# First unit as plain 32-bit products, weight splits one per item behind them, and a chunk's steps over more slots

## The reference

```python
mag = np.sqrt(a_re * a_re + a_im * a_im)
scale = np.minimum(mag, 0.999) / (mag + 1e-06)
for t in range(S):
    S_re, S_im = ar * S_re - ai * S_im + kv, ar * S_im + ai * S_re
    y[:, :, t] = q[:, :, t] @ S_re
x = y as (3072, 384)
h = x @ w_in;  x = (h * clip(h + 3, 0, 6) / 6) @ w_out        # first layer, d_ff 2048
h = x @ w2_in; out = (max(h, 0) + alpha * min(h, 0)) @ w2_out  # second layer
```

## Time and profile before

| | us |
|---|---|
| median of 3 runs (1019.43 to 1021.28) | 1019.67 |
| time of the profiled execution | 1020.87 |
| its span, first to last instruction | 1018.8 |
| PE busy (matmul) | 959.4 |
| DVE busy | 601.2 |
| ACT busy | 490.1 |
| POOL busy | 274.6 |

### The profile page before, as it was taken

How to read it: one execution, slowest core, us unless ns; L and a number is a source line. 1 busy time by engine, 2 the same in 40 slices (tenths; PEclk the granted TensorE clock), 3 DMA queues, 4 the chain that set the end, 5 groups by cost and what they waited for, 6 DMA issues and landing times.

```text
span 1018.8 us, 17268 instructions
## 1 busy us (share of the span) xinstructions
PE 959.4 (94%) x6594; PEld 865.3 (85%) x6594; DVE 601.2 (59%) x1090; ACT 490.1 (48%) x881; POOL 274.6 (27%) x251
## 2 busy tenths in 40 slices
PE   0787988999999999999999999999999999999997
PEld 0687888999999999999999998888888888888886
DVE  6888776768887787868872345452433433334332
ACT  7777757667686766767743443221221222212211
POOL 0012222222222222222222333333333333323332
PEclk9999999999999999999999999999999999999999
DMA  5762333343333333432321701010010010100000
GB/s 165 199 156 72 86 75 82 92 106 83 91 94 80 80 99 81 106 97 70 85 62 28 279 24 55 1 41 23 1 63 0 1 62 1 62 1 1 31 1 32
DMA packets 80931, 70.50 MB, mean 69 GB/s; under 512 B 32592, under 2 KB 78160, under 8 KB 80464
## 3 DMA queue, kind: packets, MB, share of 16 engines
q1 hardware_dynamic: 80208, 68.80, 24.7%
q10 hardware_dynamic: 640, 0.59, 0.2%
HBM read 40.90 MB, written 9.44 MB: 49 GB/s over the span
## 4 chain that ended last, share of the span: by engine, by line
PE 75%; DVE 13%; issue 3%; ACT 3%; SPq 3%; DMA 1%; DVEq 0%; ACTq 0%
PE hp L1188 11%; PE hp L1189 11%; PE op L1188 11%; PE hp L1190 11%; PE op L1189 11%; PE op L1190 11%; PE yp L1176 3%; PE gp L1183 3%; DVE gated L882 2%; DVE t_phase L794 2%; SPq L395 2%; DVE t_fb L822 1%; PE gp L1155 1%; SPq L398 1%; DVE t_fb L828 1%
## 5 line engine op out<-in xcount | busy, mean ns | idle before, releaser
L517 POOL TENSOR_TENSOR g_lo<-gated,g_hi 128x384 fp32r<-128x384 f32 (+2 forms) x240 | 272.4, 1135 | 734.8 <-ACT g_hi L612 734.8
L612 ACT ACTIVATE g_hi<-gated 128x384 fp32r<-128x384 f32 (+2 forms) x240 | 129.9, 541 | 344.6 <-DVE gated L897 284.4
L893 DVE TENSOR_SCALAR gate<-hp,alpha_sb 128x512 f32<-128x512 f32 x96 | 72.1, 751 | 239.9 <-PE hp L1190 239.9
L1188 PE MATMUL hp<-x_hi,wa_hi 128*128 128x384 f32 (+1 forms) x432 | 141.9, 329 | 10.4 <-DVE gated L882 9.2
L1188 PE MATMUL op<-g_hi,wb_hi 128*128 128x384 f32 (+1 forms) x432 | 143.0, 331 | 4.3 <-POOL g_lo L517 4.3
L882 DVE SCALAR_TENSOR_TENSOR gated<-gate,hp 128x384 f32<-128x384 f32 (+1 forms) x144 | 72.9, 506 | 121.2 <-ACT gate L605 121.1
L1190 PE MATMUL hp<-x_hi,wa_lo 128*128 128x384 f32 (+1 forms) x432 | 138.7, 321 | 0.0
L1189 PE MATMUL hp<-x_lo,wa_hi 128*128 128x384 f32 (+1 forms) x432 | 138.7, 321 | 0.0
L1190 PE MATMUL op<-g_hi,wb_lo 128*128 128x384 f32 (+1 forms) x432 | 137.6, 318 | 0.0
L1189 PE MATMUL op<-g_lo,wb_hi 128*128 128x384 f32 (+1 forms) x432 | 137.5, 318 | 0.0
L605 ACT ACTIVATE gate<-hp,half 128x384 f32<-128x384 f32 (+1 forms) x144 | 77.2, 536 | 91.8 <-PE hp L1190 91.7
(11 more groups left out here) (107 smaller groups left out, 1581.6 us busy)
## 6 DMA issues: line engine op xcount, KB each, us to landing
st<-prod SPq DMA_DIRECT2D x92, 145.1 KB, 3.0
a_sb<-a_in SPq DMA_DIRECT2D x24, 288.0 KB, 4.0
qk_sb<-qk_in SPq DMA_DIRECT2D x24, 288.0 KB, 3.6
v_pad<-v_in SPq DMA_DIRECT2D x24, 192.0 KB, 3.8
x_raw<-x SPq DMA_DIRECT2D x6, 768.0 KB, 5.7
out<-out_sb SPq DMA_DIRECT2D x6, 768.0 KB, 4.1
st<-prod SPq DMA_DIRECT2D x96, 32.2 KB, 2.2
wa_raw<-w_in SPq DMA_DIRECT2D x6, 512.0 KB, 6.1
```

What stands on the lines that cost most here:

```text
L517: pool.tensor_tensor(g_lo[:, at, 0:wide], gated[:, at * UT:at * UT + wide], g_hi[:, at, 0:wide].bitcast(F32), ALU.subtract).then_inc(glo_d ...
L612: act.activation(g_hi[:, at, 0:wide], gated[:, at * UT:at * UT + wide], ACT.Copy).then_inc(ghi_done, 1)
L893: dve.tensor_scalar(gate[:, at], hp[:, n % 2, 0:wide], 0.0, alpha_sb[:, m:m + 1], ALU.min, ALU.mult).then_inc(gate_done, 1)
L1188: pe.matmul(acc, lhs[0], rhs[0], start=start, stop=False)
```

## The change

In unit 0 `hidden` and `output` are one plain 32-bit product in place of three in fp32r. They read the landed weights (`wa_raw`, `wb_raw`), `x_raw` (which ACT's `x_high` now writes for chunks 0 and 1) and `gated`. So `high` and `low` are gone for items 0 to 15, and `x_low` for chunks 0 and 1. The 24 splits are one per slot, in slots 3 to 26; a DVE split waits until unit 0 has read its block. The letters of steps and the lengths are new: chunks 2 to 8 have a plan SHORT, with product, mask and output steps in slots of their own, the others a plan LONG, close to the one before; `copy_ends` stands behind `high`, and DVE's `gate1` stands ahead of `forward` where b is not with a.

```diff
-STEPS = {5: (0, 1, 1, 2, 3, 3, 4), 6: (0, 1, 1, 2, 3, 3, 4), 7: (0, 1, 1, 3, 4, 5, 6)}
+SHORT = {6: ("a", "bf", "cdo", "egv", "hij", "kl"), 7: ("a", "bf", "cdo", "egv", "hi", "j", "kl")}
+LONG = {5: ("ab", "cdefg", "ov", "hij", "kl"), 6: ("ab", "cdefg", "ov", "hij", "kl", "")}
-LENGTHS = (7, 6, 7, 7, 6, 6, 7, 5, 5, 5, 6, 5, 5, 6, 5, 5, 6, 5, 5, 6, 5, 6)
+LENGTHS = (6, 6, 6, 6, 7, 7, 7) + 4 * (5, 5, 6) + (5, 6, 6)
-W_EARLY = 8
-W_ITEM = 2
+W_ITEM = 3
-    return range(W_EARLY + W_ITEM * n, min(W_EARLY + W_ITEM * (n + 1), len(W_ORDER)))
+    return range(max(0, n - W_ITEM), min(max(0, n + 1 - W_ITEM), len(W_ORDER)))
...
     # SP
-                if "D" in steps:
+                if "g" in steps:
                     if c1 is not None:
                         stack(c1)
...
     # ACT
-                if "A" in steps:
+                if "a" in steps:
                     if keeps:
                         copy_k(c0, 0)
                     if c1 is not None:
                         waves(c1)
-                        copy_ends(c1)
-                if "B" in steps:
+                if "c" in steps:
                     if keeps:
                         copy_k(c0, 1)
                     if c2 is not None:
                         logs(c2)
...
-                high(n + GSTEP)
+                if n + GSTEP >= MT_FF:
+                    high(n + GSTEP)
+                if "b" in steps and c1 is not None:
+                    copy_ends(c1)
                 for w in splits_at(n):
                     split_w(w)
...
     # DVE
+                if "a" in steps and c1 is not None:
                     phases(c1)
                     fractions(c1)
+                    if "b" in steps:
+                        forward(c1)
+                gate1(n + GSTEP)
+                if "b" in steps and "a" not in steps and c1 is not None:
                     forward(c1)
-                gate1(n + GSTEP)
-                if "B" in steps and c1 is not None:
+                if "c" in steps and c1 is not None:
                     backward(c1)
-                if "C" in steps:
-                    if c1 is not None:
-                        product(c1, 0)
+                if "d" in steps and c1 is not None:
+                    with_qk(c1)
+                if "e" in steps and c1 is not None:
+                    product(c1, 0)
+                if "f" in steps:
                     mask(c0, 0)
                     mask(c0, 1)
-                    if c1 is not None:
-                        product(c1, 1)
+                if "g" in steps and c1 is not None:
+                    product(c1, 1)
...
     # PE
+                    if u == 0:
+                        pe.wait_ge(wa_landed[2 * k + m * P//W_DMA], 16)
+                        mm = pe.matmul(hp[:, n % 2, 0:wide], wa_raw[:, at], x_raw[:, u, k, 0:wide], start=k == 0,
+                                       stop=k == KT_DM - 1)
+                    else:
+                        mm = three(...)
...
+                    if u == 0:
+                        mm = pe.matmul(op[:, j, 0:wide], wb_raw[:, at], gated[:, n % GRING * UT:n % GRING * UT + wide],
+                                       start=m == 0, stop=m == MT_FF - 1)
+                    else:
+                        mm = three(...)
...
-                if "D" in steps:
+                if "o" in steps:
                     outputs(c0)
                     if keeps:
                         new_state(c0)
```

More of the change, by code:

```diff
@@ L74 @@
 B_BLOCKS = [(1, n) for n in range(NWI)]
-W_ORDER = (A_BLOCKS[0] + B_BLOCKS[0:1] + A_BLOCKS[1] + B_BLOCKS[1:4] + A_BLOCKS[2] + B_BLOCKS[4:6] + A_BLOCKS[3]
-           + B_BLOCKS[6:])
-W_EARLY = 8
-W_ITEM = 2
+W_ORDER = [b for q in range(NQ) for b in A_BLOCKS[q] + B_BLOCKS[(0, 1, 3, 6)[q]:(1, 3, 6, NWI)[q]]]
+W_ITEM = 3
 NRP = 12
@@ L120, in places @@
         items = items_of(s)
-        for i, n in enumerate(items):
-            yield ("".join(x for x, at in zip("ABCDEFG", STEPS[len(items)]) if at == i), n, chunk_at(s), chunk_at(s + 1),
+        plan = (SHORT if width(items[-1] // MT_FF) == FIRST * CH else LONG)[len(items)]
+        for steps, n in zip(plan, items):
+            yield (steps, n, chunk_at(s), chunk_at(s + 1),
                    chunk_at(s + 2), chunk_at(s + 3))
@@ L443, in _ @@
                         load_qk(c2)
-                if "F" in steps and c1 is not None:
+                if "j" in steps and c1 is not None:
                     load_v(c1)
-                if "G" in steps:
+                if "k" in steps:
                     c4 = chunk_at(c0 + 4)
@@ L529, in _ @@
                                pattern=[[1, ROWS2]], channel_multiplier=-1).then_inc(masks_set, 1)
-            for n in range(NT):
+            for n in range(MT_FF, NT):
                 low(n)
@@ L598, in x_high @@
                 need(act, h_done, (u - 1) * MT_FF)
[L599 removed]
+                to = x_hi if u > 0 else x_raw
+                act.activation(to[:, u % 2, :, x_cols(c)], y_place(c), ACT.Copy).then_inc(xhi_done, 1)
             def gate_of(n):
@@ L640, in _ @@
             act.wait_ge(consts_set, 1)
[L641 to L645, removed]
             def decay_parts(c):
@@ L679, in _ @@
             x_high(1)
-            split_some(W_EARLY - 4)
             inverses(3)
-            for n in range(2):
-                gate_of(n)
-                high(n)
+            gate_of(0)
+            gate_of(1)
             squares(4)
@@ L707, in _ @@
                         logs(c2)
-                if "D" in steps and c2 is not None:
+                if "v" in steps and c2 is not None:
                     inverses(c2)
-                if "E" in steps:
+                if "h" in steps:
                     x_high(c0)
-                if "F" in steps and c3 is not None:
+                if "j" in steps and c3 is not None:
                     squares(c3)
-                if "G" in steps and c2 is not None:
+                if "k" in steps and c2 is not None:
                     angle(c2)
-                high(n + GSTEP)
+                if n + GSTEP >= MT_FF:
+                    high(n + GSTEP)
+                if "b" in steps and c1 is not None:
+                    copy_ends(c1)
                 for w in splits_at(n):
@@ L877, in gate1 @@
                 dve.wait_ge(gate_done, n + 1)
-                need(dve, glo_done, n - GRING + 1)
+                if n >= GRING:
+                    if n - GRING < MT_FF:
+                        dve.wait_ge(o_done, n - GRING + 1)
+                    else:
+                        dve.wait_ge(glo_done, rounded(n - GRING))
                 wide = width(n // MT_FF)
@@ L924, in _ @@
             dve.wait_ge(consts_set, 2)
[L925 to L929, removed]
             def decay_parts(c):
@@ L944, in _ @@
             backward(0)
+            with_qk(0)
             dve.wait_ge(pads_set, 3)
-            products(0)
+            product(0, 0)
+            product(0, 1)
             decay_parts(1)
@@ L952, in _ @@
             backward(1)
-            products(1)
+            with_qk(1)
+            product(1, 0)
+            product(1, 1)
             dve.wait_ge(masks_set, 4)
@@ L967, in _ @@
             backward(2)
-            split_some(2)
-            x_low(1)
-            products(2)
+            with_qk(2)
+            product(2, 0)
+            product(2, 1)
             gate1(0)
-            split_some(2)
             gate1(1)
             state(1)
-            split_some(2)
             decay_parts(3)
@@ L1007, in _ @@
                     ratio(c2)
[L1008 to L1013, removed]
+                if "k" in steps and c2 is not None:
+                    lost(c2)
+                    decays(c2)
+                if "l" in steps and c3 is not None:
+                    mags(c3)
                 for w in splits_at(n):
@@ L1152, in score @@
                 elif c >= FIRST:
-                    pe.wait_ge(x_done, c)
+                    need(pe, x_done, c - FIRST)
                 for h in range(G4 * k, G4 * k + G4):
@@ L1262, in _ @@
                 first_half(n)
-                if "A" in steps:
+                if "a" in steps:
                     score(c0, 1)
                 second_half(n)
-                if "A" in steps and keeps:
+                if "a" in steps and keeps:
                     turn_k(c0, 1)
-                if "D" in steps:
+                if "o" in steps:
                     outputs(c0)
```

61 lines of the change are left out of this document (32 added, 29 removed).

## The result

The changed kernel takes 1028.6 us (median of 4, 1026.65 to 1029.72) against 1019.55: a ratio of 1.0085 with an interval of 1.0064 to 1.0105. It is slower. The profiled execution took 1026.65, its span is 1024.7; it is the fastest of the four, so its span is only 5.9 us longer than the one before, and the medians lie 9 apart.

The account below looks back on a forecast made before the run. Ahead of 231 us chains between engines taking turns bound the kernel, behind it PE. Terms: -1.0 - 0.3 + 2.6 = +1.3, +4.8 with the halfway transfer, plus 4 for the clock, +9 on the median; predicted 1028, range 1004 to 1040.

Parts of the forecast that it names:

- the loop by the stack: Chunks 2 to 8: each score waits for the later product and its twelve stack DMAs; 1028.7 us, chance 0.55.
- Rival 3: The stack is in time because DVE reaches the product by 9.5 us behind the score; -17, 1003 us, chance 0.25.
- the seven stretches: Score to score, chunks 2 to 9: 166.8 us against 167.1 with the shortest transfer, 0.5 more each halfway to the longer.
- the start: Ahead of the first items: removed splits start hidden(0) 1.3 us earlier and bring the score of chunk 2 1.0 earlier.
- The loop's first part: From a score to the end of the next chunk's product: 12.8 us without splits, where it was 8.73 before.
- the clock term: PE's waits at the scores of chunks 3 to 9 lower its clock: 4 us more than before, from 0 to 10.
- From product to score: From the product's end to the score, twelve DMA issues on one queue: 10.4 us at shortest, 10.9 taken as halfway.
- The 32-bit record: PE's plain 32-bit products in unit 0: 0.231 us per record of 256 columns, 10 us more work over 32 half slots.
- the upper bound of 0.231: A 256-column 32-bit record costs at most twice a 128-column score record; 0.231 us taken, as for 512 fp32r columns.
- The other reading of the prediction: Weight loads set the score's 0.11 us records, so 32-bit records cost 0.12; the forecast falls by some 3 us.
- The slot left over: 45 slots instead of 46 ahead of chunk 9's score; the remaining one goes to the PE-bound part, +2.6 us.
- the signs that I named: Waits on `st` of 15 to 25 us in seven pieces, near zero on `gated` and `scores`, chunk 9's score near 234.

Follow-up runs that it names:

- the compact plan: The changed kernel with the steps of chunks 2 to 8 laid as before the change, all else as changed: 1017.2 us, 1018.8 when timed again.
- the three-slot plan: The changed kernel with forward in the first slot, backward and masks in the second, the product halves in the third and fourth: 1020.6 us.
- the product one slot earlier: The changed kernel with product(c1, 0) of chunks 2 to 8 moved to the end of the third slot, ahead of the fourth slot's gate: 1020.9 us.
- both together: The changed kernel with product(c1, 0) moved to the third slot and two of twelve stack DMAs issued from ACT's queue: 1020.3 us.
- two DMAs on ACT: The changed kernel with two of the twelve stack DMAs of chunks 3 to 9 issued from ACT's queue: 1020.7 us.
- the plan alone: The kernel before the change with only the new plan and lengths, products in fp32r and splits as before: 1033.0 us.

## Why the prediction was right

**The result.** Forecast 1028, measured 1028.6, by the likeliest case, the loop by the stack. That the loop is what makes the change slower is shown from both ends: a shorter way to the product gives 7.7 us back, a shorter stack 7.9, and the old plan 11.4, each with fewer waits on `st` (17.2, 10.3 and 1.1 us in place of 20.1). Rival 3 (the stack in time, 1003) is out. It also failed where it was allowed to happen: with the waits on `st` gone, the compact plan is at 1017 to 1019, since the waits on `gated` that it took for removed come back.

**Luck in the number.** The terms add up to +8.8 us, and the pair of rows that can be compared has +5.9: +7.4 in the seven stretches (forecast +7.2), -1.7 at the start (-1.0), +0.2 behind the score of chunk 9 (+2.6). The 3 us between this and the medians lie in executions of which there are no rows. And the +7.2 itself comes out of two errors of over 6 us that cancel, told next.

**The loop's first part.** The working gave 12.8 us without splits; chunk 8 has 12.7, and the step named as the late one, ACT's gate behind `logs`, is the one that DVE waits for. With splits and in unit 0 it gave 13.8 to 14.0; chunk 2 has 14.0 (62.20 to 76.20), but chunks 3 to 7 have 15.7, 16.7, 15.6, 15.4 and 14.3. The sum over seven is 104.4 where the working has 94.0.

**The clock.** That excess of 10.4 us is what the clock term was for, and the term was too small. The working is made of rows of chunk 7, whose stretch of before has PEclk 1.00, so it holds no time at the lower level at all; I then added only what the change would have more than before, 4 us. With the clock at 1.2 or 2.4 GHz, 1 minus PEclk, doubled, times the length of a stretch is its time at 1.2: 3.6, 5.8, 8.8, 5.5 and 3.4 us, 27 in all, in just the five stretches whose score comes behind a wait of 2.0 us or more. In the three stretches of before that had any it is some 14. Of the 27, 20 lie between a score and the end of the product (PEclk 0.89, 0.90, 0.86, 0.81 and 0.88 there, and 1.00 in chunks 2 and 8), and PE is busy in that part without a gap in all but 0.2 us.

What it cost can be read in three ways. Half of the 20 us is 10.2, the most that it can be, and nearly the excess. PE's busy time against the compact plan gives 6.7 us for 23.6 more at half rate. And of the twelve executions of the three-slot plan the five with a mean granted clock of 0.984 or 0.985 took 1022.1 in the median and the seven with 0.991 to 0.995 took 1018.2: 3.9 us for some 17 more at half rate. One place has the full price: in chunk 2 of "the product one slot earlier" and of "both together" the plan up to the product is the same and PE has the same 129 matmuls, and it is 15.8 us with PEclk 0.80 behind a wait of 3.2 us, and 12.8 with 1.00 behind one of 0.3; 3.0 us for 6.3 at half rate.

So the step that was mis-sized is this term: 4 us where PE's busy time tells of 7 to 8 for the 27 us. What the other 3 us of the excess are is open; chunk 4 has `leave` of unit 0 on ACT, 0.8 us, and no run held the clock alone. Against the kernel before, PE is idle for 3.0 us more in the seven stretches (20.5 and 17.5) and busy for 4.4 more. How much of the 4.4 is the clock, with 13.6 us more at half rate, and how much the longer 32-bit slots less the one slot that is gone, these rows don't separate.

**From product to score.** I took 10.9 us, "halfway" between the two seen before (halfway from 10.4 to 11.7 is 11.05); measured are 9.8 four times, 10.1 once and 10.4 twice, in sum 70.0 in place of 76.3. This error hides the one above: 104.4 + 70.0 = 174.5 by the unrounded rows, 94.0 + 76.3 + 4 = 174.3 forecast.

**The 32-bit record.** 0.216 us, near the upper bound of 0.231 and far from 0.12. So a record of 256 columns costs nearly twice one in fp32r (0.12). The Trainium skill gives a true 32-bit product four passes through the array ("FP8 and Floating Point Precision", TensorE Precision Notes). The trace agrees: 0.432 us a product is 1037 clocks at 2.4 GHz, four for each of 256 columns. The other reading of the prediction, by the Trainium skill's rule that a weight load takes a time set by its columns ("TensorE: Matmul & The Clock Gate", LDWEIGHTS), went with the lower bound of 0.12, which is out. The half slots of unit 0 are 7 us more work for PE where I had 10; the experiment that has only them and the splits is level with the kernel before, so this size hardly mattered to the time.

**The slot left over.** I took 2.6 us for it. From the score of chunk 9 on, with one slot more, it is 788.0 us against 787.8: 0.2. The term counted the work of the slot and not the idle time that it could fill: before, PE was idle for 1.6 us between 231 and 544 (busy for 311.6 of 313.2), 1.3 of it on `st`, and in as long a part behind the score of chunk 9 of the change it has no gap (313.3 of 313.3). That gave back 1.6 of the 2.4; where the last 0.8 went, no run tells.

**The start.** -1.4 us at the first item where I had -1.3, and -1.7 at the score of chunk 2 where I had -1.0.

**The signs.** Of the signs that I named, the waits on `st` (20.1 us in seven pieces) and the end of the waits on `gated` and `scores` are there. The score of chunk 9 came at 236.7 (forecast near 234), and from a score to the end of the product it is 12.7 to 16.7 us where I had 12 to 14, the excess told above.

## What to carry to other kernels

When engines walk one list of slots in order, count the loop from a result to its next use through every queue head on the way, and not the work in each slot: here two gates more on the way to one product cost more than the waits that the spreading removed. The longest share of one engine between two gates is the other side of it, since the partner's in-order queue stands behind the gate: with 8.1 us in one slot in place of 6.3 the kernel was 18 us slower. Ask of every wait that you move what TensorE's clock does behind it: PE is idle for only 3 us more in the seven stretches of the change than before, and has twice the time at half rate. And where two edits each give 8 us by shortening one loop, don't expect 16: look at which wait is second.

## What the runs showed of the hardware

The time of a many-part transfer was mostly that of its issues on one queue: in the seven stacks of the change twelve DMAs took 7.7 to 8.3 us to issue, and the score started 2.0 us behind the last issue. With the last two, of 145 KB each, on another queue it was 1.9 us shorter, 1.2 by the issues and 0.7 by the time from the last issue to the score. That the 0.7 comes from small parts, which land 1.9 us behind their issue and not 2.9, now standing last is argued.

Waits of 2.0 to 6.5 us of PE, one per chunk, went with the lower clock behind them in five of five stretches of the change; waits of 1.5 and 0.9 did not. It is no fixed rule: in "two DMAs on ACT" a wait of 2.5 us ahead of chunk 2, and in "the plan alone" one of 2.8 ahead of chunk 8, had the full clock behind them, and in "both together" the stretch behind a wait of 1.2 (chunk 4) has 0.87. The time at half rate was twice that of before, 27 us against 14.

A plain 32-bit product of 256 columns took two records of 0.216 us each at 2.4 GHz, and three fp32r products of the same size 0.36 us.
